# Loading the first expert's weights five attention steps earlier, and dropping a semaphore between VectorE and GpSimd

## What is computed

```python
scores = scale * q @ k.T                       # per batch and head, 576 x 576
thresh = max(scores) - tau
scores = where(scores >= thresh, scores, -1e9)
attn = exp(scores - max(scores));  attn /= sum(attn) + 1e-9
x = attn @ v                                   # 2304 tokens x 512
e = argmax(x @ w_gate + modality_bias[modality_id])
x = gate_w * (relu(x @ w1[e]) @ w2[e])         # w1 512 x 1024, w2 1024 x 512 per expert
h = x @ w_in
out = (h * tanh(softplus(h))) @ w_out
```

## Time and profile before

| | us |
|---|---|
| median of 3 runs | 945.03 |
| lowest, highest | 944.0, 946.19 |
| time of the profiled execution | 945.03 |
| its span in the trace | 943.4 |

### The profile page before, as it was taken

The page is one execution under the profiler, slowest core; times in us unless marked ns, Lnnn a source line. Parts: engine busy times, 40 slices in busy tenths (PEclk is TensorE's granted clock), DMA queues, the critical chain, the costliest instruction groups (busy, mean ns, idle before and its releaser), DMA issues.

```text
span 943.4 us, 19421 instructions
## 1 busy us (share of the span) xinstructions
PE 918.3 (97%) x6976; PEld 771.4 (82%) x6977; DVE 672.4 (71%) x1227; ACT 508.6 (54%) x987; POOL 474.7 (50%) x560
## 2 busy tenths in 40 slices
PE   6999999999999999999999989999999999999996
PEld 5777777777778788888877978899889898889985
DVE  6999999999965411111153898888888788788793
ACT  5777777878752422222255465545555455455552
POOL 5222234556522763000000586777786777777884
PEclk9999999999999999999999999999999999999999
DMA  4131236333115563111234100101001000000000
GB/s 130 53 102 52 82 123 233 143 109 102 50 58 197 158 257 81 47 36 47 70 131 175 45 1 1 35 34 35 23 12 35 34 1 1 33 1 1 34 1 34
DMA packets 21937, 65.97 MB, mean 70 GB/s; under 512 B 3552, under 2 KB 3552, under 8 KB 21600
## 3 DMA queue, kind: packets, MB, share of 16 engines
q1 hardware_dynamic: 14512, 39.90, 12.6%
q0 software_dynamic: 4896, 20.00, 6.2%
q10 hardware_dynamic: 2448, 5.01, 1.7%
HBM read 46.63 MB, written 18.27 MB: 69 GB/s over the span
## 4 chain that ended last, share of the span: by engine, by line
PE 61%; DVE 5%; issue 4%; ACT 1%; ACTq 1%; POOL 0%; DVEq 0%; POOLq 0%
PE psum L1421 6%; PE psum L1423 6%; PE psum L1422 6%; PE psum L1413 6%; PE psum L1411 6%; PE psum L1412 6%; PE psum L1084 3%; PE psum L1086 3%; PE psum L1085 3%; PE psum L1111 3%; PE psum L1113 3%; PE psum L1112 3%; DVE rr L1533 2%; PE psum L1095 2%; PE psum L1070 1%
## 5 line engine op out<-in xcount | busy, mean ns | idle before, releaser
L1533 DVE RECIPROCAL rr<-rr 128x384 f32<-128x384 f32 x96 | 244.1, 2542 | 9.9 <-ACT rr L1481 9.9
L1359 POOL TENSOR_TENSOR uu<-uu,ex 128x384 f32<-128x384 f32 x96 | 97.4, 1014 | 101.2 <-ACT uu L1475 101.2
L579 ACT ACTIVATE prob<-ssb,smin 128x576 f32<-128x576 f32 x144 | 111.6, 776 | 63.1 <-DVE ssb L701 63.0
L1411 PE MATMUL psum<-x2T_hi,w_in_hi 128*128 128x384 f32 x384 | 131.2, 342 | 4.3 <-DVE gg L1539 2.7
L1413 PE MATMUL psum<-x2T_hi,w_in_lo 128*128 128x384 f32 x384 | 129.8, 338 | 0.0
L1412 PE MATMUL psum<-x2T_lo,w_in_hi 128*128 128x384 f32 x384 | 129.3, 337 | 0.0
L1165 DVE TENSOR_TENSOR hT_lo<-psum,hT_hi 128x512 fp32r<-128x512 f32 x38 | 26.3, 691 | 140.3 <-ACT hT_hi L1142 140.3
L701 DVE TENSOR_SCALAR_CACHE_REDUCE ssb<-psum,tauk 128x576 f32<-128x576 f32 x144 | 112.1, 811 | 13.1 <-PE psum L424 10.4
L1481 ACT ACTIVATE rr<-uu 128x384 f32<-128x384 f32 x96 | 50.5, 526 | 118.7 <-POOL uu L1359 118.7
L1421 PE MATMUL psum<-w_hi,g_hi 128*128 128x512 f32 x288 | 114.3, 397 | 0.1
L1422 PE MATMUL psum<-w_lo,g_hi 128*128 128x512 f32 x288 | 114.0, 396 | 0.0
(11 more groups left out here) (210 smaller groups left out, 2118.9 us busy)
## 6 DMA issues: line engine op xcount, KB each, us to landing
qk<-in_qk_dram SPq DMA_DIRECT2D x15, 640.0 KB, 4.1
vsb<-in_v_dram SPq DMA_DIRECT2D x16, 512.0 KB, 3.6
xrow<-xs ACTq DMA_DIRECT2D x17, 288.0 KB, 2.9
ys<-ysb SPq DMA_DIRECT2D x19, 257.0 KB, 3.0
stage<-in_w_in_dram POOLq DMA_DIRECT2D x16, 256.0 KB, 4.4
wa<-in_wa_dram SPq DMA_DIRECT2D x8, 512.0 KB, 7.6
wb<-in_wb_dram SPq DMA_DIRECT2D x8, 512.0 KB, 10.3
xs<-zrow SPq DMA_DIRECT2D x11, 288.0 KB, 2.8
```

The costliest lines, as they stand in the source:

```text
L579: act.activation(prob[:, n % 3, cols], ssb[:, w, cols], ACT.Exp, bias=smin[:, w, h:h + 1], scale=-1.0).then_inc(exp_done, 1)
L1411: pe.matmul(bank_of(n), w_in_hi[:, k, cols], xT_hi[w][:, k], start=(k == 0), stop=False)
L1533: dve.reciprocal(rr[:, n % 4], rr[:, n % 4]).then_inc(r_done, 1)
```

## The change

`LOAD_AT` goes from 45 to 40: `load_lead` moves five iterations forward in POOL's queue. There it stands between scatter 1 and scatter 2 of batch 0. `SPLIT_AT` becomes 46 to 54 and 61 to 67: the pieces of iterations 68 to 71 move to 46 to 49, and with them ACT's casts and, one iteration later, POOL's subtractions. The semaphore `quiet` goes: POOL's wait ahead of each of the 16 subtractions, and DVE's 16 increments.

```diff
-LOAD_AT = ROUTE + RANK + 13
+LOAD_AT = ROUTE + RANK + 8
...
-SPLIT_AT = [c for c in range(LOAD_AT + 5, NS) if not SCATTER_AT <= (c - ROUTE) % PER <= SCATTER_AT + TT][:2 * PIECES]
+SPLIT_AT = [c for c in range(LOAD_AT + 6, NS) if not SCATTER_AT <= (c - ROUTE) % PER <= SCATTER_AT + TT][:2 * PIECES]
...
-    quiet = sem("quiet")
...
             pool.wait_ge(lead_hi_done, i + 1)
-            pool.wait_ge(quiet, i + 1)
             low = pool.tensor_tensor(lo, raw, hi.bitcast(F32), ALU.subtract)
...
-            if c - 1 in SPLIT_AT:
-                dve.sem_inc(quiet, 1)
```

## The result

| | us |
|---|---|
| kernel before, median of 4 runs of this comparison | 945.61 (944.0 to 946.52) |
| changed kernel, median of 4 runs | 951.79 (951.71 to 952.17) |
| changed / before | 1.0068, 95% interval 1.005 to 1.0086 |
| profiled execution of the changed kernel, and its span | 950.58, 948.9 |

The change makes the kernel slower by 6.2 us, 0.68%. The prediction was 947.2 us with a range to 949.6: the direction was right, and the stall that it built on is there with nearly the size given. Three more things came on top in this profile: DVE operations that POOL's subtractions hold up (a term that the prediction had as a gain), a stretch at half clock behind the stall, and a pause of PE late in attention.

The account below looks back on a forecast made before the run. In attention, the first 268 us, DVE and PE were taken to pass the lead to each other. Terms +0.05 + 2.4 - 0.3 = +2.15 us on span 943.4, with 1.63 around it, gave 947.2 us; range 944.6 to 949.6.

Parts of the forecast that it names:

- Part 1: POOL's queue, iteration 40: the moved loads make block 41's limit and DVE's mask late; +0.05 us (0 to +0.5).
- Part 2: Scatters 2 to 4 queue behind the loads; DVE's normalise of block 41 waits; +2.4 us (+1.2 to +4.0).
- Rival A: No stall at normalise, scatters landing before 157.6 us: 944.8 us, not slower; chance 0.15.
- rival B: Longer stall, last scatter landing 5.8 us after wb: +6.1 in place of +2.4, 950.9 us; chance 0.05.
- Part 3: Without quiet, subtractions slip in behind DVE's masks and two mask collisions of 0.22 us go; -0.3 us (-0.44 to 0).
- Rival C: Guard needed: subtractions take the port before the second mask in six iterations, 5.7 us, 952.9 with the stall; chance 0.04.
- Part 4: Four subtractions move from iterations 69 to 72 to 47 to 50, like 67 to 70 one batch later; 0 us.

Follow-up runs that it names:

- wb_late: Kernel before with pieces moved and wa loaded in iteration 40, but wb in 45 behind the scatters; quiet stays: 945.18 us, ratio 0.9996.
- act_loads: Kernel before with loads and pieces moved, quiet kept, both loads started from ACT's queue in iteration 40: 947.21 us, ratio 1.0007.
- after: The changed kernel in its first comparison with the kernel before: 951.79 us, ratio 1.0068.
- no_quiet: Kernel before with only the semaphore quiet removed; loads and pieces stay where they were: 947.69 us, ratio 1.0025.
- bare_spread: Kernel before without quiet, loads unmoved, SPLIT_AT chosen so no subtraction stands before small routing operations or behind a scatter: 943.25 us, ratio 0.9984.
- move_only: Kernel before with only the loads and pieces moved as in the change; quiet stays: 949.61 us, ratio 1.0038.
- after_again: The changed kernel run once more, unchanged, against the kernel before: 953.04 us, ratio 1.0082.
- pe_filled: The changed kernel plus four unused matmuls on PE ahead of the output rows of block 42, to fill the stall: 950.63 us, ratio 1.0047.
- spread: Kernel before with only SPLIT_AT changed, leaving out iterations whose subtraction ran into a mask; quiet and loads untouched: 943.86 us, ratio 0.998.
- after_third: The changed kernel run again, unchanged, against the kernel before: 951.31 us, ratio 1.0063.
- pe_filled5: The changed kernel plus five unused matmuls on PE ahead of the output rows of block 42: 949.87 us, ratio 1.0054.
- spread_again: Kernel before with only SPLIT_AT changed to avoid mask collisions, quiet and loads untouched, measured a second time: 943.76 us, ratio 0.9986.

## Why the prediction was wrong

**Part 1, the limit of block 41: the size was right (0.05 predicted, nothing measured), the lateness behind it didn't come.** The limit stood at 139.74, 0.3 us later than before once the 1.5 to 1.6 us between the two executions are taken off, and took 0.49 us where the earlier trace rows had 0.77; no step moves by more than 0.1 us between 7 and 46. The loads left sooner than I had worked out: wb's issue is at 139.16, and on the clock of this execution, 1.5 us ahead of the other's, 142.91 - 1.5 = 141.4 had been expected. The 1.26 us of waiting ahead of wa did not come, and scatter 1 was 1 us sooner.

**Part 2, the scatters queue behind the loads: right, +2.4 us predicted and +2.40 measured.** wb_late and act_loads show that the place in the queue decides between a stall and none. The agreement to the digit is luck, though: wb landed 1.4 us sooner than worked out (154.9 against 157.8 - 1.5 = 156.3) and the scatters needed 3.5 us behind it in place of 2.1. The two errors cancel. The 1.8 us for the scatters had assumed 410 GB/s to the end; in the trace the DMA engines move at most 155 GB/s, mostly 50 to 110, from 155.9 on. In the six profiles with this queue order the wait was 2.3 to 3.5 us. Rival A (no stall) and rival B (5.8 us behind wb) are out.

The sentence that the prediction cites from "DMA: Bandwidth & Descriptors" of the Trainium skill is written there of the queues of SP and ACT, and the section adds that completion is not in order per issuing engine; it doesn't say by itself that scatters on POOL's queue land behind wb. The runs show that: the first packet of scatter 2 at 152.4, wb landed at 154.9, the last scatter at 158.1.

**What was missed behind part 2: the clock.** The prediction let PE stand for 2 us and charged only the standing. The price of what comes next is +0.80 to +0.81 us at step 48 in each of the changed kernel's three profiles. The clock row of the page of before reads 9 throughout, and the prediction took that for a clock granted in full. Read more finely it could have warned: the stretch 13 to 19 us has a granted clock of 0.72, around two waits of PE of 1.15 and 0.68 us (in the trace of after the same stretch reads 1.00).

**Part 3, `quiet` goes: the step that failed.** The prediction asked where the subtraction would stand relative to the masks, and that part is right: it slipped in behind the second mask in iterations 48, 53, 63, 66 and 68 with 1.87 us each, and two masks of 1.02 became 0.81 (-0.22 each). The error is the sentence that "the next copies from PSUM ... don't need the port". No copy from PSUM was held; but between mask and copy DVE has routing work, and some of it does need the port. Once the subtraction had it, a 0.17 us COPY took 1.23. The iterations with an `rsum`, which the prediction passed over with "0.3 us sooner or the same", are the dearest: 52 and 72 cost 1.0 us each, because 0.3 us sooner is just ahead of the COPY. Measured alone (no_quiet) the term is +2.2 us in the time and +3.1 in the steps, in place of -0.3. The step that failed is that the list of what `quiet` protects was drawn up from its most frequent user, the mask, and not from all DVE operations in the reach of a subtraction. bare_spread is the proof: no guard, no such operation in reach, no cost. **Rival C** had the right idea, that the guard was needed, but named the wrong victims (six masks at 0.95 us), and got a chance of 0.04.

The page "SBUF — State Buffer" of the Trainium skill, section "Who interferes with whom", names among the DVE instructions that can take the shared port `copy`, `cast` and `tensor_scalar`, besides those with two SBUF inputs, and says that `tensor_reduce` on trn2 never contends. The traces agree: COPY 0.17 to 1.23, TENSOR_SCALAR 0.17 to 0.66, TENSOR_TENSOR 0.19 to 0.90, while the TENSOR_REDUCE at the head of the routing work of iteration 53 kept its 0.18. The prediction read from that page the rule on order and not the list beside it.

**Part 4, four subtractions move: 0 predicted.** With `quiet` kept the new places cost 0.34 us (move_only, wb_late and act_loads alike). Without it, iteration 48 costs +0.71, and leaving iteration 72 saves the 1.01 us of no_quiet. The argument that 47 to 50 are like 67 to 70 one batch later held: 68 costs 0.60 as well. What it left out is what happens there without `quiet`. It also missed that `quiet` ran iteration 48's subtraction into a mask (1.01 us) as it had that of 68.

**The sum.** +0.05 + 2.4 - 0.3 had given 947.2. With +2.2 for part 3 and 0.8 for the clock it is 945.6 + 2.4 + 2.2 + 0.8 = 951.0 on this comparison's median (951.5 with the 2.7 of the account's port lines). The 951.8 measured leaves 0.8 us or less. The 0.8 for the clock is read from profiles, not measured alone.

**What stays open.** PE's pause of about 1.1 us in iteration 77 is in the profiles of after, after_again, pe_filled and act_loads and not in those of before, no_quiet, move_only, wb_late, spread, after_third, pe_filled5, spread_again and bare_spread. It follows neither the stall nor `quiet`, and the profile names nothing on the core that causes it. It may be the 0.8 us that is left; no run settles it. Nor was it settled how often the half clock comes behind the stall: it did in three of three profiles of the changed kernel and not in the one of move_only. And move_only's median lies 1.4 us above what its profile accounts for.

## What to carry to other kernels

A semaphore that keeps two engines off a shared port protects every instruction in its reach: before it goes, list all of the other engine's operations that use the port within the length of the guarded one, the tiny ones most of all, since here a 0.17 us operation took 1.2 us. Small transfers that somebody waits for don't belong behind megabytes in the same queue; either the big one leaves after them or on another engine's queue, and here either took the 4 us away. The first is the safer: wb_late had 4 us to spare and act_loads 0.7, because the megabytes delay the small transfers from another queue as well. Where a change makes PE stand in the middle of a kernel, look at the clock behind the place too: here 0.8 us came on top of a wait of 2.4.

## What the runs showed of the hardware

- A DVE operation on 128 x 5 values can be held for the whole of a 128 x 512 operation of POOL: 0.17 against 1.23 us (COPY), 0.17 against 0.66 (TENSOR_SCALAR), 0.19 against 0.90 (TENSOR_TENSOR with both inputs in SBUF), each ending within 0.06 us of POOL's. A TENSOR_REDUCE and operations that read PSUM in the same places kept their times.
- The last scatter's last packet ended 5.4 us after its issue began with no loads under way, 9.2 us with 4 MB under way on another queue (act_loads), and 11.8 and 11.9 us behind the 4 MB on the same queue (move_only, the changed kernel). The queue held the scatters back by 2.6 us on top of the 3.8 of sharing, and with both DVE waited 2.3 to 3.5 us.
- Shortly after PE had waited 1.85, 1.95 and 2.08 us, the granted clock went from full to half for 3.4 us in the three profiled executions of the changed kernel; in one of move_only, after a wait of 1.88 us, it did not, and with PE's stall filled by five matmuls it did not. With four (waits of 1.11 and 0.57 us) it did. Over all timed runs the mean granted clock was 0.9938 with the stall unfilled and 0.9967 with it filled.
- The price of a half clock was small beside its length: 3.4 us at half, +0.8 us of time. That DVE sets the pace in most of these steps is the likely reason.
